# Top-32 attention and two feed-forward layers in fp32: an unrolled slot plan, Prelu as the mask, V stationary

## The reference

```python
def _attn_ref(q, k, v):            # batch 4, heads 8, seq 576, head_dim 64
    scores = scale * np.matmul(q, k.transpose(0, 1, 3, 2))
    kth = np.partition(scores, -top_k, axis=-1)[..., -top_k:-top_k + 1]   # top_k = 32
    scores = np.where(scores >= kth, scores, -1000000000.0)
    attn = np.exp(scores - np.max(scores, axis=-1, keepdims=True))
    attn = attn / (np.sum(attn, axis=-1, keepdims=True) + 1e-09)
    return np.matmul(attn, v)

def _moe_ref(x, w_in, w_out):      # 2304 tokens, 512 -> 2048 -> 512
    h = x @ w_in
    return (h - np.tanh(h)) @ w_out

def _moe2_ref(x, w_in, w_out):
    h = x @ w_in
    return np.where(h > 0.0, h, np.exp(np.minimum(h, 0.0)) - 1.0) @ w_out
```

## Time and profile before

| | |
|---|---|
| median of 3 runs | 1284.62 us (1283.78 to 1285.82) |
| profiled execution, its own span | 1281.9 us |
| instructions | 23141 |
| busy | PE 1203.8, PEld 1039.2, DVE 896.5, ACT 702.2, POOL 790.3 us |
| mean granted TensorE clock | 0.980 |
| chain that ended last | PE 71%, issue 12%, DVE 6%, ACT 5%, POOL 4% |
| DMA | 56.81 MB, mean 44 GB/s |

### The profile page before, as it was taken

How to read it: one execution, slowest core, us unless ns; L and a number is a source line. 1 busy time by engine, 2 the same in 40 slices (tenths; PEclk the granted TensorE clock), 3 DMA queues, 4 the chain that set the end, 5 groups by cost and what they waited for, 6 DMA issues and landing times.

```text
span 1281.9 us, 23141 instructions
## 1 busy us (share of the span) xinstructions
PE 1203.8 (94%) x6784; PEld 1039.2 (81%) x6784; DVE 896.5 (70%) x1870; ACT 702.2 (55%) x1534; POOL 790.3 (62%) x579
## 2 busy tenths in 40 slices
PE   3678999999998999999999999999999999999997
PEld 2667887888887888888888888788888888888887
DVE  7999999999999999999999995015532222222221
ACT  5667777766776766777766765345432222222221
POOL 4898888888987888988888986332222222222221
PEclk9679999999999999999999999999999999999999
DMA  6410022000022100022000000504001001010000
GB/s 201 168 56 13 20 62 75 30 21 22 23 68 64 32 21 21 25 66 68 28 26 13 21 11 12 188 12 170 1 1 66 1 1 65 0 50 1 1 33 17
DMA packets 46420, 56.81 MB, mean 44 GB/s; under 512 B 13296, under 2 KB 28656, under 8 KB 45808
## 3 DMA queue, kind: packets, MB, share of 16 engines
q1 hardware_dynamic: 46320, 55.59, 13.7%
HBM read 45.61 MB, written 9.96 MB: 43 GB/s over the span
## 4 chain that ended last, share of the span: by engine, by line
PE 71%; issue 12%; DVE 6%; ACT 5%; POOL 4%; DVEq 0%; DMA 0%; ACTq 0%; POOLq 0%; SPq 0%
PE ps L683 15%; PE ps L728 15%; PE ps L611 11%; PE ps L626 10%; PE ps L598 9%; PE ps L579 4%; PE ps L563 2%; PE ps L564 2%; PE ps L653 2%; DVE best L973 1%; POOL keep L1104 1%; DVE work L1005 1%; DVE best L964 1%; PE ps L580 1%; ACT kT_hi_over_lo L755 1%
## 5 line engine op out<-in xcount | busy, mean ns | idle before, releaser
L1104 POOL TENSOR_SCALAR keep<-scores,best 128x576 f32<-128x576 f32 x144 | 253.6, 1761 | 58.3 <-DVE best L964 55.9
L1148 POOL TENSOR_TENSOR elu_lo<-elu_h,elu_hi 128x512 fp32r<-128x512 f32 x72 | 92.9, 1290 | 305.7 <-ACT elu_hi L755 305.7
L598 PEld LDWEIGHTS ps<-v_and_one,weights_T 128*128 128x128 f32 (+1 forms) x1440 | 183.5, 198 | 56.0 <-issue 49.3
L598 PE MATMUL ps<-v_and_one,weights_T 128*128 128x129 f32 (+2 forms) x1440 | 196.1, 285 | 34.9 <-ACT x L865 33.0
L1110 POOL TENSOR_TENSOR kept_weights<-work,keep 128x576 f32<-128x576 f32 x144 | 205.9, 1430 | 26.8 <-POOL keep L1104 17.8
L964 DVE MAX8 best<-work 128x8 f32<-128x576 f32 x288 | 213.8, 742 | 0.2
L1043 DVE TENSOR_SCALAR exp_h<-exp_h 128x512 f32<-128x512 f32 x72 | 30.7, 427 | 239.9 <-ACT exp_h L907 239.9
L755 ACT ACTIVATE weights_T<-ps 128x512 f32<-128x512 f32 (+1 forms) x288 | 115.1, 433 | 118.6 <-PE ps L580 105.1
L907 ACT ACTIVATE exp_h<-ps 128x512 f32<-128x512 f32 x72 | 43.1, 598 | 194.3 <-PE ps L683 194.3
L821 ACT ACTIVATE work<-scores,exp_bias 128x576 f32<-128x576 f32 x144 | 111.6, 775 | 24.4 <-DVE best L964 24.0
L563 PE MATMUL ps<-kT_hi_over_lo,qT_hi 128*128 128x288 f32 (+1 forms) x320 | 106.1, 347 | 20.1 <-DVE kT_hi_over_lo L937 15.5
(11 more groups left out here) (83 smaller groups left out, 2880.7 us busy)
## 6 DMA issues: line engine op xcount, KB each, us to landing
kT_raw<-kT SPq DMA_DIRECT2D x64, 144.0 KB, 2.8
w_in_raw<-w_in SPq DMA_DIRECT2D x8, 1024.0 KB, 7.5
w_out_raw<-w_out SPq DMA_DIRECT2D x8, 1024.0 KB, 5.5
qT_raw<-qT SPq DMA_DIRECT2D x64, 96.0 KB, 2.5
ffn_rows<-act SPq DMA_DIRECT2D x18, 256.0 KB, 2.1
v_and_one<-v SPq DMA_DIRECT2D x16, 256.0 KB, 2.7
rows<-ffn_rows SPq DMA_DIRECT2D x4, 1024.0 KB, 6.5
out<-out_rows SPq DMA_DIRECT2D x16, 256.0 KB, 2.4
```

The costliest lines, as they stand in the source:

```text
L598: mm = pe.matmul(ps[:, B_OUT, 0:2 * D + 1], pt[0:k, c, :], rhs, start=(c == 0), stop=(c == FULL))
L1104: nc.gpsimd.tensor_scalar(keep[:, :], sc[:, i, :], best[:, i, TOP - 1:TOP], None, ALU.is_ge).then_inc(kept, 1)
```

## The change

All engines are rewritten as one plain list of slots, unrolled at build time, s = -1 to 169. A unit is a number t; tail units follow tile 0 of each batch. What an engine does in slot s:

- TensorE: `attend` for the pair that ended with unit s-3, scores of s+1, one chunk of the first layer, transposes of unit s-2, the second layer of the chunk before.
- ScalarE: Prelu and exponential of unit s-2 (with the activation split between), copy of scores s+1, copies of x, splits, tanh of the chunk, and last the copies of the turned weights of unit s-2.
- VectorE: the seven searches of units s and s-1, the reciprocal for unit s-2.
- GpSimd: activation low part, sum + eps of unit s-2, splits, normalisation of unit s-2, weight splits, the difference, the biases of unit s-1.

The mask is made without a comparison: Prelu of (score - threshold) with slope 1e30 leaves the kept ones as they are and sends the others far below zero, where the exponential gives 0. The exponential also gives the sum. The weights are normalised in place before they are transposed. V is stationary (64 columns of it for each half of a pair), the weights move, and the result is x already transposed. The first layer has 128 columns of `w_in` stationary and 256 tokens moving, so its activations need no transposing either. Groups are of 256 tokens, 16 chunks each; nine groups take slots 24 to 167. The second feed-forward layer keeps its order, without loops.

```diff
-                            nc.vector.tensor_tensor(lo, raw, hi, ALU.subtract).then_inc(w_split_dve, 1)
-                        nc.gpsimd.tensor_scalar(keep[:, :], sc[:, i, :], best[:, i, TOP - 1:TOP], None, ALU.is_ge
-                                                ).then_inc(kept, 1)
-                        nc.gpsimd.tensor_tensor(kept_w[:, :], wk[:, i, :], keep[:, :], ALU.mult).then_inc(masked, 1)
-                    for n, (l, r) in enumerate(((xt_hi, win_hi), (xt_hi, win_lo), (xt_lo, win_hi))):
-                        mm = pe.matmul(ps[:, B_H + fb % 2, :], l[:, kc, :], r[:, kc, ws],
+STEEP = 1.0e30
+    QRING = 3
+        first = max(last_unit_of[tiles[g * GN + GN - 1]] + READY, h_slot[-1] + 1 if h_slot else 0)
+        h_slot += range(first, first + FC)
+    y_slot = [s + 1 for s in h_slot]
+        W_FROM = 5
+        w_slot = {W_FROM + i: (2 * i, 2 * i + 1) for i in range(CPB * len(W_ORDER) // 2)}
+            def attend(u):
...
                 for c in range(FULL + 1):
+                    k = P if c < FULL else REST
+                    for half in (0, 1):
+                        values = vals[0:k, c, u.pair, :] if c < FULL else vals_rest[0:k, u.pair, :]
+                        if u.tail:
+                            weights = pt[0:k, u.t % 2, c, half * D:(half + 1) * D]
+                        else:
+                            weights = pt[0:k, (u.t - 1 + half) % 2, c, :]
+                        mm = pe.matmul(ps[half * D:(half + 1) * D, B_OUT, cols], values[:, half * D:(half + 1) * D],
+                                       weights, start=(c == 0), stop=(c == FULL))
                 mm.then_inc(attended, 1)
+            def h_step(i):
...
+                for kc in range(KC):
+                    for n, (l, r) in enumerate(((win_hi, xt_hi), (win_lo, xt_hi), (win_hi, xt_lo))):
+                        mm = pe.matmul(ps[:, B_H + i % 2, 0:N], l[:, kc, fs], r[:, kc, ring:ring + N],
                                        start=(kc == 0 and n == 0), stop=(kc == KC - 1 and n == 2))
+                mm.then_inc(h_done, 1)
...
+            for s in range(-1, LAST + 1):
+                done, old, new = unit(s - 3), unit(s - 2), unit(s + 1)
+                if done and done.ends_pair:
+                    attend(done)
+                if new:
+                    scores(new)
+                if s in h_in:
+                    h_step(h_in[s])
+                if old:
+                    turn_weights(old)
+                if s in y_in:
+                    y_step(y_in[s])
...
+            def cut_scores(u):
+                sc_e.wait_ge(biased, u.t + 1)
+                nc.scalar.activation(sc[:, u.t % 4, :], sc[:, u.t % 4, :], ACT.Prelu, bias=bias[:, u.t % 2, 0:1],
+                                     scale=1.0, alpha=STEEP).then_inc(cut, 1)
+
+            def exp_scores(u):
+                sc_e.wait_ge(cut, u.t + 1)
+                after(sc_e, summed, u.t - 1)
+                nc.scalar.activation(sc[:, u.t % 4, :], sc[:, u.t % 4, :], ACT.Exp, bias=bias[:, u.t % 2, 1:2],
+                                     scale=1.0, accum_out=sums[:, u.t % 2:u.t % 2 + 1]).then_inc(exped, 1)
...
+            for s in range(-1, LAST + 1):
+                new, old, done = unit(s + 1), unit(s - 2), unit(s - 3)
+                if old:
+                    cut_scores(old)
+                if s - 1 in h_in:
+                    g_high_part(h_in[s - 1])
+                if old:
+                    exp_scores(old)
+                if new:
+                    copy_scores(new)
...
+                for n in w_slot.get(s, ()):
+                    w_high_part(n)
+                if s in h_in:
+                    tanh_step(h_in[s])
+                if old:
+                    copy_turned(old)
...
+            for s in range(-1, LAST + 1):
+                new, old, exped_u = unit(s), unit(s - 1), unit(s - 2)
+                if new:
+                    top(new, 0)
+                if old:
+                    top(old, 2)
+                if new:
+                    drop(new, 0)
+                if old:
+                    drop(old, 2)
+                if exped_u:
+                    invert(exped_u)
...
+                if new:
+                    top(new, 1)
+                if old:
+                    top(old, 3)
+                if new:
+                    drop(new, 1)
...
+            def norm(u):
+                po.wait_ge(inverted, u.t + 1)
+                w = sc[:, u.t % 4, :]
+                nc.gpsimd.tensor_scalar(w, w, rinv[:, u.t % 2:u.t % 2 + 1], 1.0, ALU.mult, ALU.mult).then_inc(normed, 1)
...
+            for s in range(-1, LAST + 1):
+                old, exped_u, done = unit(s - 1), unit(s - 2), unit(s - 4)
+                if s - 1 in h_in:
+                    g_low_part(h_in[s - 1])
+                if exped_u:
+                    sum_eps(exped_u)
+                if s - 1 in k_slot:
+                    k_low_part(*k_slot[s - 1], s)
...
+                        x_low_part(tile)
...
+                        q_low_part(n)
+                if exped_u:
+                    norm(exped_u)
+                for n in w_slot.get(s, ()):
+                    w_low_part(n)
...
+                if s in h_in:
+                    difference(h_in[s])
+                if old:
+                    biases(old)
```

1172 lines of the change are left out of this document (483 added, 689 removed).

## The result

The changed kernel takes **1503.5 us** (median of four runs, 1501.2 to 1505.7) against 1284.2 for the kernel before: ratio **1.171**, 95% interval 1.170 to 1.173. I had forecast 1397 and a range up to 1450. The direction and the mechanism hold, the size does not: the span is 1502.3 us where my sum gave 1394.

What follows compares the result with a forecast made beforehand. One unit's serial chain through the engines and uneven TensorE slots were taken to set the time: 13 + 43 + 98 + 750 + 82 + 408 = 1394 us of span, plus 2.7, 1397; range 1300 to 1450.

Steps and rivals of the forecast that it cites:

- The waits named in advance: Predicted signs: VectorE's reciprocal waits on GpSimd, GpSimd's normalisation on VectorE, and ScalarE's Prelu follows straight on its copies.
- The uneven slots: Middle slots: the pair-ending one set by TensorE at 6.07 us, the other by the unit's chain at 5.81.
- the attention product at 2.2 us: TensorE, per pair: 20 instructions at 0.11 us, the two halves one after the other; bounds 1.1 and 2.2.
- this rival: Attention halves overlap on TensorE: slots of 4.97 and 5.64 us, total 1334, or 1298 with a cheaper normalisation; chance 0.26.
- chain plus single additions, 5.94 us: Slots 24 to 143: mean of 6.07 (TensorE) and 5.81 (chain 4.85 + 0.57 + 0.39), 713 us over 120.
- 20 us for x, 17 for keys (half hidden) and 0.39 a slot for queries: Splits in the 120 slots: 15 of x at 1.3, 24 of keys at 1.4, query split 0.39 beyond the reciprocal.
- 6.1 us a slot: Slots 5 to 20, two GpSimd weight splits between normalisation and biases: 2.31 + 0.82 + 2.5 + 0.28 + 0.2; 16 make 98.
- 8 slots of about 5.3: Slots without FFN or weight splits among 0 to 23: 4.66, half a query split and 0.5 for the clock; 43 us.
- the chain of 4.85: One unit's serial steps, Prelu through normalisation, transposes and copies, as a slot's least period; 4.66 without the activation split.
- Unrolling itself I cost at nothing: Second FFN: unrolling adds no time, as TensorE in that stage has 100% of its time already; stage 408 us.
- the clock case: Rival: TensorE's granted clock falls to its lower level in a quarter of the 120 slots, +75 us, 1470; chance 0.10.
- the overlap rival: Attention halves on different partitions run side by side on TensorE, 120 slots of 5.3 us, 1334 in all; chance 0.26.

Runs made afterwards that it cites:

- later: Changed kernel with unit transposes and the copies of the turned weights one slot later: 1386.4 us, ratio 1.079.
- norm_short: Changed kernel with GpSimd's normalisation cut to the first 64 of 576 columns of a unit: 1474.2 us.
- same_half: Changed kernel with both halves of an attention product written to the same 64 partitions: 1575.6 us.
- splits_behind: Changed kernel with GpSimd's low parts of keys and x behind the normalisation, those of queries behind the next unit's biases: 1424.6 us, ratio 1.111.
- weights_spread: Changed kernel with the eight first-layer weight loads issued one a slot in slots 0 to 7, not all ahead of the loop: 1489.7 us.
- y_second_row: Changed kernel with the first FFN's second output row block given its own buffer and its copy moved next to the first one's: 1480.7 us.
- filler_matmuls: Changed kernel with five or eight unread fp32 products ahead of each unit's transposes, none in full slots: 1489.0 us.
- later_k_copy: Changed kernel with transposes one slot later and five more moves, plus upper key copies on GpSimd, copy and split ending its slot: 1295.8 us, ratio 1.009.
- later_behind: Changed kernel with all moves so far, plus ScalarE's key/query high parts behind copy and tanh, GpSimd's x/query low parts behind normalisation: 1289.7 us, ratio 1.0043.

## Why the prediction was wrong

**What held.** That the kernel gets slower, and why: all steps of unit s-2 stand one after the other in one slot. `later` shows it (-117 us, slots at VectorE's 4.88). The waits named in advance are there: reciprocals wait 209.8 us in total for GpSimd's sum, TensorE's transposes 206.8 for the normalisation; Prelu follows on the copies with 50.8 us of waiting in all 144 units. The uneven slots are there too, the pair-ending one TensorE's, the other the chain's; `norm_short` and `same_half` show both sides (-29 and +72). The prices of the single operations on ScalarE, VectorE and GpSimd were right within 0.1 us.

**The step that I had chosen wrongly: the attention product at 2.2 us.** The halves overlap and the 20 instructions take 1.39 us. I had given this rival 0.26 and 1334 us. By the nearest row of before, a transpose followed by a wide matmul, I chose against it; that row has no two instructions on different columns with 64 each, and says nothing on the case. The Trainium skill has the rule ("TensorE: Matmul & The Clock Gate", Part 3: matmuls of few stationary columns on distinct column groups run concurrently), and this trace agrees, 0.064 against 0.118 us apart. This mistake hid the larger one: without it the forecast would have been near 1334, 169 us too low. The rival's slots, 4.97 and 5.64 us, came out at 5.52 and 5.66: in TensorE's slot the second layer takes 1.56 where I had 1.36, attention 1.39 for 1.1, scores 0.63 for 0.52. That the sum was only 108 us short is luck: too dear an attention covered a part of what was missing elsewhere.

**The step that failed: a slot's length as chain plus single additions, 5.94 us for each of 120.** The clean slots are shorter (5.6). But slots are rarely clean, and what is added to the chain I had counted too low: the 120 slots took 797.6 us for 750, slots 0 to 23 184.7 for 144, and the rest of the first FFN 89.3 for 79. It shows in four places:
- *GpSimd's splits between sum and normalisation.* I had 20 us for x, 17 for keys (half hidden) and 0.39 a slot for queries, as if they came one at a time. They come together at a batch end, one behind the other, and hold the normalisation back by 3.76 us: `splits_behind` gives 79 us back by order alone, 36 of them at the three batch ends.
- *Weight splits in slots 5 to 20.* I had 6.1 us a slot; they average 7.2 (115.5 us in 16). The 6.1 is right where only GpSimd's 2.5 us count. In the slots of 7.9 attention, scores and ScalarE's high parts (0.63 each) stand ahead of GpSimd's split, and I had none of them in that slot's chain. The order of GpSimd alone is worth 29, 17.5 of them here.
- *The start.* "8 slots of about 5.3" passes over SyncE's queue: the weights' eight loads stand ahead of query group 3, one slot takes 24.8 us. My sum has no term for that queue. 14 us by `weights_spread`.
- *The second row block.* Its copy stands behind the copies of the turned weights, and TensorE asks for both banks at once: 1.42 us of waiting at each of seven group ends and 2.20 at an eighth. I had no term for it. 23 us by `y_second_row`. At 1086.9 us, at the last group's end, the DMA itself (2.0 us) stands between the two copies, and ScalarE waits 2.12 us for it.

These prices overlap (a wait that one edit takes away may be another's cover), so they are not summed to 169. One figure of the sum doesn't follow from its own terms: without the activation split the chain of 4.85 would be 4.85 - 0.33 = 4.52, not 4.66. Over 8 slots that is 1 us.

**A smaller miss: the second FFN, 416.2 us for 408.** 6.5 us of it is that the same matmuls follow each other more slowly than before (2.80 and 2.76 us for twelve, against 2.72), the other 1.7 us its beginning. "Unrolling itself I cost at nothing" was a term put at nothing without a row for it. Whether unrolling, the placement of the buffers or something else slows these matmuls, no run separates.

**The clock.** I had the lower level as a rival with a quarter of the slots. Its mean is 0.56 from 100 to 180 us, 0.87 at a batch end and 1.00 in the clean slots from 455 to 478. It fell after waits (5.10 us ahead of 488.85, a second one of 1.42 at 424.44), though not after each (1.61 at 462.07). `filler_matmuls` raises the mean over the span from 0.91 to 0.94 and gains 14 us, 7 of them at the batch ends: a share of the loss, not its cause. How much of each price in the four places above is the clock's is not shown; the attention at 142 us, 1.98 us for what takes 1.09, says that it is not nothing.

**The range.** Its upper end was half of the clock case, as if the extras of the chain could only be as large as I had them. Every doubtful term of a latency chain errs to the same side (what was overlooked is always an addition), and I had let the overlap rival pull the range down instead.

**What stays open.** Around a batch end a slot takes 5.8 us even in the best version, where neither order of GpSimd's or ScalarE's queue helps, and 6.5 in `splits_behind`. Whether the tails' own matmuls, ScalarE's key parts or the clock there decide was not separated. Nor is it known why the second FFN's matmuls follow each other more slowly in the rewritten kernels (2.80 and 2.76 us in `later`, `same_half`, `splits_behind`, `later_k_copy` and `later_behind` too).

## What to carry to other kernels

When steps of one item are drawn together into one slot, write down for each queue everything that stands between two links of that item's chain, slot by slot, above all in the slots where rare work falls together; busy shares (GpSimd: 41%) say nothing of it. Put what nobody waits for soon behind the links, or give the item one slot more: here the one was worth 79 us and the other 117, with the same instructions. Read the DMA queue in the same way: a load that isn't needed for 5 slots should not stand ahead of one that is needed in the next. When a price is bounded from both sides by rows of another kind of instruction, keep both cases in full to the end of the sum.

## What the runs showed of the hardware

- Two fp32 products of 64 stationary columns on different column ranges: 0.064 us an instruction at 128 moving columns, against 0.118 on one range (`same_half`).
- GpSimd's TENSOR_SCALAR with a per-partition factor: 318 ns at 64 elements, 749 at 576, so 0.84 ns an element over 0.26 us. The comparison of the same 576 elements took 1761 ns: the operation matters more than the number of inputs. The Trainium skill's rule for one input ("GPSIMD Engine Reference", Engine selection: roughly line-rate) comes near for the first (VectorE's MAX8 over 576 takes 744 to 754 ns here) and not for the second.
- The sum output of an exponential is an instruction of its own, 189 ns (ACTIVATION_READ_ACCUMULATOR), which the next link waits for.
- Prelu with a pointer bias costs what the exponential does (773 and 766 ns) and needs no second table load.
- GpSimd's copy of 64x576 with rounding took 0.67 us beside 1.42 for the subtraction of the same size (`later_k_copy`).
